# An MLP over 768 tokens in float32 parts: blocks of 512 and 256 tokens in place of 384 and 384

## What is computed

```python
state = alpha[t] * state + outer(k[t], v[t]);  y[t] = q[t] @ state      # 8 heads of 48, gives x (B, 768, 384)
u = x + real(fft(fft(x, tokens), features)); un = normalised(u); x = u + relu(un @ w_ch1) @ w_ch2
h = relu(x.transpose(0, 2, 1) @ w_tok1) @ w_tok2                        # mixes tokens, 768 -> 256 -> 768
u = x + h.transpose(0, 2, 1)
h2 = relu(u @ moe2_w_ch1) @ moe2_w_ch2                                  # the second MLP, 384 -> 1536 -> 384
out = u + h2
```

## Time and profile before

| | us |
|---|---|
| median of three runs | 991.17 |
| lowest and highest | 989.49, 991.56 |
| the profiled execution, its own time | 993.23 |
| its span, first to last instruction | 991.4 |
| TensorE busy | 941.7 |
| VectorE busy | 458.8 |
| ScalarE busy | 253.1 |
| GpSimd busy | 172.8 |
| mean granted TensorE clock | 0.986 |

### The profile page before, as it was taken

How to read it: one execution, slowest core, us unless ns; L and a number is a source line. 1 busy time by engine, 2 the same in 40 slices (tenths; PEclk the granted TensorE clock), 3 DMA queues, 4 the chain that set the end, 5 groups by cost and what they waited for, 6 DMA issues and landing times.

```text
span 991.4 us, 16182 instructions
## 1 busy us (share of the span) xinstructions
PE 941.7 (95%) x5716; PEld 894.5 (90%) x5716; DVE 458.8 (46%) x1099; ACT 253.1 (26%) x641; POOL 172.8 (17%) x282
## 2 busy tenths in 40 slices
PE   4688899999899998899998999999999999999998
PEld 3567899998899998899997999899999999999998
DVE  5466765655855646855556222522142233314222
ACT  2323332224322223322233422321122112211111
POOL 3481222110212111211101331200020010002000
PEclk9999999999899999899998999999999999999999
DMA  8824002323022213023001600200010001000000
GB/s 239 247 49 94 3 5 45 72 49 74 1 49 43 53 27 74 2 49 73 1 11 53 217 24 20 101 1 24 24 48 0 24 24 48 24 0 24 0 24 24
DMA packets 14250, 48.70 MB, mean 49 GB/s; under 512 B 1664, under 2 KB 5888, under 8 KB 12480
## 3 DMA queue, kind: packets, MB, share of 16 engines
q1 hardware_dynamic: 13056, 41.88, 16.0%
q10 hardware_dynamic: 544, 2.36, 1.3%
q0 software_dynamic: 576, 3.55, 1.1%
HBM read 38.35 MB, written 9.44 MB: 48 GB/s over the span
## 4 chain that ended last, share of the span: by engine, by line
PE 85%; DVE 5%; DMA 4%; issue 3%; ACT 1%; POOL 1%; SPq 0%; ACTq 0%; DVEq 0%; POOLq 0%
PE bank L1092 17%; PE bank L1094 15%; PE bank L1093 15%; PE heads L1094 7%; PE heads L1093 7%; PE heads L1092 7%; PE bank L1133 4%; PE heads L1108 4%; PE bank L1137 2%; DMA vt<-v 2%; PE bank L1144 2%; DMA raw_a<-w_ch 1%; PE bank L1099 1%; PE heads L1202 1%; PE heads L1307 1%
## 5 line engine op out<-in xcount | busy, mean ns | idle before, releaser
L937 DVE SCALAR_TENSOR_TENSOR hl<-bank,hh 128x384 fp32r<-128x384 f32 x192 | 106.9, 557 | 333.4 <-ACT hh L572 333.4
L572 ACT ACTIVATE hh<-bank 128x384 fp32r<-128x384 f32 x192 | 94.4, 492 | 306.0 <-PE bank L1094 306.0
L1092 PE MATMUL bank<-nh,w1h 128*128 128x384 f32 x288 | 108.3, 376 | 2.3 <-DVE nl L895 2.1
L1094 PE MATMUL bank<-nh,w1l 128*128 128x384 f32 x288 | 100.0, 347 | 0.0
L1093 PE MATMUL bank<-nl,w1h 128*128 128x384 f32 x288 | 100.0, 347 | 0.0
L1092 PE MATMUL bank<-u2h,w3h 128*128 128x384 f32 x288 | 97.9, 340 | 0.5 <-DVE u2l L1048 0.2
L1094 PE MATMUL bank<-u2h,w3l 128*128 128x384 f32 x288 | 97.4, 338 | 0.0
L1093 PE MATMUL bank<-u2l,w3h 128*128 128x384 f32 x288 | 97.0, 337 | 0.0
L424 POOL TENSOR_TENSOR qkap<-qkap,suf 112x128 f32<-112x128 f32 x96 | 39.8, 414 | 306.1 <-DVE suf L703 299.7
L466 POOL TENSOR_TENSOR u<-u,x2l 128x384 f32<-128x384 f32 x24 | 23.6, 1012 | 288.8 <-DVE u L1069 288.8
L499 ACT ACTIVATE dec<-st,suf 112x96 f32<-112x96 f32 x80 | 30.1, 377 | 166.9 <-DVE st L685 106.8
(11 more groups left out here) (185 smaller groups left out, 2017.2 us busy)
## 6 DMA issues: line engine op xcount, KB each, us to landing
qkap<-qka SPq DMA_DIRECT2D x26, 432.0 KB, 7.0
raw_a<-w_ch SPq DMA_DIRECT2D x6, 768.0 KB, 13.1
mid<-u SPq DMA_DIRECT2D x8, 576.0 KB, 2.9
raw_b<-w_ch SPq DMA_DIRECT2D x6, 768.0 KB, 5.5
xr<-mid SPq DMA_DIRECT2D x8, 576.0 KB, 4.1
out<-u SPq DMA_DIRECT2D x8, 576.0 KB, 2.7
vt<-v SPq DMA_DIRECT2D x14, 288.0 KB, 7.4
qkap<-qka ACTq DMA_DIRECT2D x4, 432.0 KB, 8.1
```

The costliest lines, as they stand in the source:

```text
L572: act.activation(hh[:, s % 4, :], bank[s % 2][:, 0:HALF], ACT.Relu).then_inc(s_hhi, 1)
L937: dve.scalar_tensor_tensor(out=hl[:, s % 4, :], in0=bank[s % 2][:, 0:HALF], scalar=0.0, in1=hh[:, s % 4, :].bitcast(F32), op0=ALU.max, op1 ...
L1092: pe.matmul(out_ap, wh, rh, start=first, stop=False)
L1094: return pe.matmul(out_ap, wl, rh, start=False, stop=last)
```

## The change

The second MLP takes a batch's 768 tokens as a block of 512 (tiles 0 to 3) and one of 256 (tiles 4 and 5). `wide_in` has 512 or 256 columns for each of its nine matmuls; `wide_out` has four or two tiles of three matmuls. A fourth accumulator, bank 5, comes in. `turn(3)` also uses bank 5, and the first block now includes tile 3, so `turn(3)` and its split stand ahead of the MLP and TensorE waits for four split tiles. Turns 4 and 5 follow after `wide_in(1)` and `(2)`. The hidden slices have a new place in SBUF, as wide as the larger block.

```diff
+WIDE = 512
...
+    wide_h = sb("wide_h", [P, 4, WIDE], o_a + 4 * MB, F32R)
+    wide_l = sb("wide_l", [P, 4, WIDE], o_a + 4 * MB + 4 * WIDE * 4, F32R)
+    assert o_a + 4 * MB + 8 * WIDE * 4 <= o_small + 2 * SPLIT_W * 4
...
-    ACC = bank[2:5]
+    ACC = bank[2:6]
+    BLOCKS = (slice(0, WIDE), slice(WIDE, S))
+    TILES = ((0, 1, 2, 3), (4, 5))
...
+            def hidden_wide(bi, s):
+                n = (WIDE, S - WIDE)[s // NF]
+                act.wait_ge(s_hp, bi * MLP + s + 1)
+                act.wait_ge(s_l2, bi * MLP + s - 3 + L2_PRIMED)
+                act.activation(wide_h[:, s % 4, 0:n], bank[s % 2][:, 0:n], ACT.Relu).then_inc(s_hhi, 1)
...
                 token_mix(b)
-                for t in range(3):
+                for t in range(4):
                     split_u2(b, t)
                 for s in range(MLP):
-                    hidden(b + B, s)
-                    if s in (2, 3, 4):
-                        split_u2(b, s + 1)
+                    hidden_wide(b + B, s)
+                    if s in (2, 3):
+                        split_u2(b, s + 2)
...
+            def hidden_wide(bi, s):
+                n = (WIDE, S - WIDE)[s // NF]
+                dve.wait_ge(s_hhi, bi * MLP + s + 1)
+                dve.scalar_tensor_tensor(out=wide_l[:, s % 4, 0:n], in0=bank[s % 2][:, 0:n], scalar=0.0,
+                                         in1=wide_h[:, s % 4, 0:n].bitcast(F32), op0=ALU.max, op1=ALU.subtract
+                                         ).then_inc(s_hlo, 1)
+
             def mlp2_sum(b, blk):
-                for t in range(3):
-                    sums_done(b + B, blk, t)
-                    dve.tensor_tensor(u2[:, 3 * blk + t, :], ACC[t][:, 0:DM], u2[:, 3 * blk + t, :], ALU.add
-                                      ).then_inc(s_fin, 1)
+                for i, t in enumerate(TILES[blk]):
+                    if t in (3, 5):
+                        dve.wait_ge(s_l2, (b + B) * MLP + NF * (blk + 1) + L2_PRIMED)
+                    else:
+                        dve.wait_ge(s_acc, (b + B) * 4 + 3 * blk + i + 1)
+                    dve.tensor_tensor(u2[:, t, :], ACC[i][:, 0:DM], u2[:, t, :], ALU.add).then_inc(s_fin, 1)
             def phase_b(b, more):
                 for i in range(2):
...
                     dve.wait_ge(s_mix, b * NC + t + 1)
                     dve.tensor_tensor(u2[:, t, :], bank[MIX_BANKS[t]][:, 0:DM], x2h[:, t, :].bitcast(F32), ALU.add
                                       ).then_inc(s_half, 1)
-                    for done in {3: (0,), 4: (1, 2)}.get(t, ()):
+                    for done in {3: (0,), 4: (1, 2), 5: (3,)}.get(t, ()):
                         split_u2(b, done)
                 for s in range(MLP + 2):
                     if s < MLP:
-                        hidden(b + B, s)
-                    if s in (2, 3, 4):
-                        split_u2(b, s + 1)
+                        hidden_wide(b + B, s)
+                    if s in (2, 3):
+                        split_u2(b, s + 2)
                     if more and s in (7, 11):
                         split_x2(b + 1, s // 11)
                     if s == NF + 1:
...
                 mm.then_inc(s_l2, 1)
+            def wide_in(bi, s):
+                blk, f = s // NF, s % NF
+                if s >= 2:
+                    pe.wait_ge(s_hlo, bi * MLP + s - 1)
+                m, cols = slice(f * P, (f + 1) * P), BLOCKS[blk]
+                n = cols.stop - cols.start
+                for k in range(KT):
+                    mm = three(bank[s % 2][:, 0:n], w3h[:, k, m], w3l[:, k, m], u2h[:, k, cols], u2l[:, k, cols],
+                               k == 0, k == KT - 1)
+                return mm
+
+            def wide_out(bi, s, base):
+
+                blk, f = s // NF, s % NF
+                pe.wait_ge(s_hlo, bi * MLP + s + 1)
+                for i in range(len(TILES[blk])):
+                    if s == NF:
+                        pe.wait_ge(s_fin, base + i + 1)
+                    m = slice(i * P, (i + 1) * P)
+                    mm = three(ACC[i][:, 0:DM], wide_h[:, s % 4, m], wide_l[:, s % 4, m], w4h[:, f, :], w4l[:, f, :],
+                               f == 0, f == NF - 1)
+                    if f == NF - 1 and i < len(TILES[blk]) - 1:
+                        mm.then_inc(s_acc, 1)
+                mm.then_inc(s_l2, 1)
+
+
             pe.wait_ge(s_const, 64)
             pe.wait_ge(s_zero, 6)
             attn_turn(0, 0).then_inc(s_krT, 1)
...
                     if t == 4:
                         turn(1)
                         turn(2)
-                pe.wait_ge(s_ulo, b * NC + 3)
+                turn(3)
+                pe.wait_ge(s_ulo, b * NC + 4)
                 for s in range(MLP + 2):
                     if s == NF:
                         pe.wait_ge(s_ulo, b * NC + NC)
                     if s < MLP:
-                        mlp_in(b + B, s, w3h, w3l, u2h, u2l).then_inc(s_hp, 1)
-                    if s in (1, 2, 3):
-                        turn(s + 2)
+                        wide_in(b + B, s).then_inc(s_hp, 1)
+                    if s in (1, 2):
+                        turn(s + 3)
                     if s >= 2:
                         if s == 2:
                             pe.wait_ge(s_half, b * NC + NC)
-                        mlp_out(b + B, s - 2, w4h, w4l, s_fin, b * NC + FIN_PRIMED)
+                        wide_out(b + B, s - 2, b * NC + FIN_PRIMED)
             with pe.Fori(0, B) as b:
                 phase_b(b)
```

## The result

Sixteen runs of each: the changed kernel's median is 993.38 us (991.24 to 997.03), that of the kernel before 991.37 us. The ratio is 1.0024, with a 95% interval of 1.0013 to 1.0034: slower by 2.4 us, between 1.3 and 3.4.

What follows compares the result with a forecast made beforehand. The prediction took TensorE's in-order instruction row to bound the kernel. Matmuls 0 plus the turn's 4.0 us, on the median of 991.17, gave 995.2 us, range 988.8 to 999.8.

Steps and rivals of the forecast that it cites:

- sign of being wrong: Second MLP: forecast wrong if the pair isn't near 351 ns, or batch distance is off 92 us with the pair as said.
- The turn ahead of the MLP: Head of each batch's MLP: TensorE starts 1.34 us later, less 0.335 inside; net 1.0 us a batch, 4.0 in all.
- The matmul pair: Hidden slices: 512 plus 256 columns cost 351 ns, like two of 384; change 0, bounds -11.4 to +4.4 us.
- Output slices, "Cost 0": Second MLP's output slices: still 216 matmuls of 384 columns a batch, so no change in time.
- What is hidden: ScalarE's and VectorE's work on hidden slices and at the block change stays covered; smallest margin 0.7 us.
- Rival 1: Hidden slices: 256-column matmuls dearer because the weight load shows; up to 4.4 us more, about 997 to 999.6 us; chance 17%.
- Rival 2: Hidden slices: 512-column matmuls cheaper, some 216 ns; 989.7 us (chance 8%), or 985 us with cheap 256 too (7%).
- Rival 3: Pause ahead of each batch's MLP lowers the clock to half: 1011 us, or 1003 at half of it; chance 4%.
- Rival 4: Head of the MLP: the added wait isn't there, or inside turns cost more than 0.335 us; 991 to 993 us; chance 6%.
- My 175.5 ns "over the whole stage": Second MLP: price of a 384-column matmul from start to start, 160 ns of columns plus 15.5 ns.

Runs made afterwards that it cites:

- turn3_early: The kernel before, blocks still 384 and 384, with only turn(3) and its split moved ahead of the MLP: 995.16 us against 991.04, ratio 1.0038.
- slices_moved_384: The kernel before with only phase B's hidden slices moved behind the weights in SBUF, still 384 wide: 989.06 us against 991.04, ratio 0.9973.
- only_high_moved: As slices_moved_384, but only the high parts at the new place, low parts at the old: 90.92 us a batch; executed once, 989.95 us.
- moving_plus_128: The kernel before with 128 bytes put in front of xh, shifting it and all tiles behind it: 985.08 us against 991.68, ratio 0.9932.

## Why the prediction held, step by step

The direction and the path held, the size did not: 4.0 us lies outside the measured 1.3 to 3.4, and the median of 993.38 is only just inside the forecast's own spread of 993 to 997. By its own sign of being wrong (a batch off 92 us with the pair as said) the forecast lacked a term: the pair is nearly as said, and a batch takes 91.61.

The single steps add up. By the distances between batches the turn alone costs 1.02 us (turn3_early) and the place alone gives back 0.45 (slices_moved_384). Together that is +0.57, and the change measures 91.61 - 91.04 = +0.57. This leaves nothing for the widths and the fourth accumulator at these addresses. No kernel had the wide slices on a multiple of 256, which would test that sum directly.

- **The turn ahead of the MLP**, 1.0 us a batch: right. Each leg was read off the old trace. The last mixing matmul to the MLP was to be 1.82 us and is 1.84; turn3_early alone gives 1.0 us a batch.
- **The matmul pair**, no change: right to 0.1 us a batch, and partly by luck. The parts were off in opposite ways, 233 ns for 512 (228.8 said) and 119 for 256 (122.2 said), and nothing in the two readings made them cancel. 0.4 us in all.
- **Output slices, "Cost 0"**: the term that was mis-sized, and the reason why 2.4 us came out instead of 4.0. I counted matmuls and columns, and passed over the new place in SBUF, which stands in the diff. In the change the output slices took 0.61 us a batch less; slices_moved_384 shows 0.56 of it by itself, and with its hidden slices 0.11 dearer a net 0.45 a batch, 1.8 in all.
- **What is hidden** stayed hidden: no wait inside the MLP is listed, none at the change of block.
- **Rival 1** (256 columns dearer) fell: they cost 119 ns. **Rival 2** (512 cheaper) fell: dearer. **Rival 3** (the clock): it stayed at full through all four pauses of the change (the nines of the page's second half). **Rival 4** (no wait): 1.2 us of waiting four times.
- The columns at 2.4 GHz plus 2.5 ns, the rule of the Trainium skill ("TensorE: Matmul & The Clock Gate", section "Wait — 56ns, not 53.3ns?"), would give 215.8 ns for 512 columns, an estimate from the page's figures. This trace doesn't agree: 233.
- My 175.5 ns "over the whole stage" was a mean over matmuls that start 168 to 182 ns apart, though all have 384 columns. That spread was the sign of something else than columns, and I didn't follow it.

## What to carry over

A block size that needs one more tile ready makes the whole pipeline wait for that tile's way through the engines; put the small block first and the wait disappears. A diff that moves a tile changes more than its code: compare the start addresses of operands before calling a matmul's price unchanged, and try a pad of 128 bytes, which gave the kernel before more (6.7 us) than the change moved. It is to be tried and not assumed: in the two kernels with wide blocks the same pad took less than 0.1 us off a batch.

## What was not expected of the hardware

- **Start addresses.** In the kernel before and its shifted forms a matmul of 384 float32 columns in the second MLP costs 173.5 to 173.8 ns from start to start within a slice where both operands start alike within 256 bytes, and 175.2 to 176.2 where they don't. Shown by six kernels for the output slices (by the sums 177.1 to 174.5 ns and back by 128 bytes, unchanged by 4608 and by a shift of everything) and by one for the hidden slices (176.4 to 174.5). The token stage, whose operands start alike in every kernel, takes 173.4 to 173.6 ns, but 174.1 in only_high_moved. What counts is open, and alike starts are not enough by themselves: in both kernels with the wide slices the output slices rose by 1 ns when only `u2h` and its neighbours moved; w2 in phase A came down only to 175.1 ns with both operands alike; and moving the high parts alone gave a third of the gain. Which accesses meet, nothing here shows.
- **The clock.** In one profile of moving_plus_128 TensorE paused for 1.9 us ahead of phase B, and the granted clock fell to half (1.2 GHz) at about 622.6 us, some 1.5 us after it had resumed; from 626.1 us on it was back at full. In the trace of before a pause of 1.7 us at the same place left it at full, and so did one of 2.0 us in slices_moved_384. So the length of the pause alone doesn't decide it. The timeline's row with the pause, the windows (the column before the last two is the granted clock), then the wait of slices_moved_384 and the window behind it:

```profile
621.11 0.45 PE L1093 MATMUL bank<-x2h,t1h 128*128 128x384 f32 x1 [1.93 <-DVE x2l L1030]
```

```profile
622.60:626.00 3.40, 3.40 (x12) 3.40 (x12) 3.08 (x5) 0.00 (x0) 0.00 (x0) 0.51 0.39 161
626.10:640.00 13.90, 13.76 (x82) 13.20 (x81) 6.45 (x12) 2.91 (x6) 5.90 (x6) 1.00 0.04 7
```

```profile
PE bank L1094 <- DVE x2l L1031: 2.0, 1, 2.0
```

```profile
620.00:624.00 4.00, 4.00 (x25) 4.00 (x24) 3.79 (x6) 0.65 (x1) 0.00 (x0) 1.00 0.31 128
```

The first token stage took 7.95 us there in place of about 6.35, which is 1.6 us in one execution that the next need not have. Phase A's half-clock stretches differ likewise from one execution to the next (6.8 and 10.2 us in the two traces under the result). With effects of 2 us it is the distance between batches that can be trusted, or many runs.
